# Eight weight slots of the second MLP combined early, sums on VectorE, and the first MLP's down layer turned to rows of tokens

## The reference

```python
kv  = einsum('bhsd,bhse->bhde', k, v); out = einsum('bhsd,bhde->bhse', q, kv)
x   = out / rms(out) * g_norm                       # 4608 tokens x 512
u   = x + real(fft(fft(x, axis=1), axis=2))         # first block
un  = (u - mean(u)) / sqrt(var(u) + 1e-6)
x   = u + relu(un @ w_ch1) @ w_ch2
u   = x + (xt @ U @ V) transposed back              # second block, rank 32
out = u + relu(u @ w_ch1b) @ w_ch2b
```

## Time and profile before

| | |
|---|---|
| median of 3 runs | 1830.46 us (1825.45 to 1831.49) |
| the profiled execution's own time | 1823.0 us |
| its span | 1820.9 us |
| TensorE matmul, busy | 1738.5 us (95%) |
| VectorE, busy | 1374.4 us (75%) |
| ScalarE, busy | 786.0 us (43%) |
| GpSimd, busy | 432.9 us (24%) |
| DMA, mean over the span | 258 GB/s |

### The profile page before, as it was taken

How to read it: one execution, slowest core, us unless ns; L and a number is a source line. 1 busy time by engine, 2 the same in 40 slices (tenths; PEclk the granted TensorE clock), 3 DMA queues, 4 the chain that set the end, 5 groups by cost and what they waited for, 6 DMA issues and landing times.

```text
span 1820.9 us, 25843 instructions
## 1 busy us (share of the span) xinstructions
PE 1738.5 (95%) x9908; PEld 1673.3 (92%) x9908; DVE 1374.4 (75%) x1631; ACT 786.0 (43%) x1126; POOL 432.9 (24%) x356
## 2 busy tenths in 40 slices
PE   6889879989999999999999999899999999999999
PEld 5667769979999999999999999799999999999999
DVE  5779987997777877867866858965956857758567
ACT  2333344554444544445444436434334434444442
POOL 2889973331120120120110013220110100100200
PEclk9889989999999999999999999999999999999999
DMA  8487557988787887887876778876766766767663
GB/s 256 161 272 250 201 201 282 370 332 283 262 303 261 283 287 258 289 286 247 297 260 232 257 246 310 333 275 231 251 236 237 257 234 242 255 231 254 224 249 128
DMA packets 123820, 470.04 MB, mean 258 GB/s; under 512 B 12274, under 2 KB 49650, under 8 KB 84019
## 3 DMA queue, kind: packets, MB, share of 16 engines
q1 hardware_dynamic: 122482, 467.21, 73.4%
q10 hardware_dynamic: 1216, 1.18, 0.2%
HBM read 389.70 MB, written 78.64 MB: 257 GB/s over the span
## 4 chain that ended last, share of the span: by engine, by line
PE 80%; DVE 12%; issue 3%; POOL 3%; DMA 2%; SPq 1%; ACT 0%; DVEq 0%; POOLq 0%; ACTq 0%
PE pair L832 12%; PE pair L834 12%; PE pair L833 12%; PE pair L849 12%; PE pair L851 12%; PE pair L850 12%; DVE t_lo L1339 2%; PE tr_ps L716 2%; PE pair L623 2%; DVE t_raw L1358 2%; DMA in_sb<-x_dram 1%; DVE w_sb L1271 1%; DMA v_sb<-v_rest 1%; DVE eo_sb L1229 1%; POOL x_sb L1528 1%
## 5 line engine op out<-in xcount | busy, mean ns | idle before, releaser
L849 PE MATMUL pair<-t_hi,w_sb 128*128 128x384 f32 x1344 | 460.4, 343 | 17.1 <-DVE t_lo L1339 16.7
L832 PE MATMUL pair<-t_hi,w_sb 128*128 128x384 f32 x1344 | 459.8, 342 | 7.0 <-DVE h_sb L1376 6.9
L851 PE MATMUL pair<-t_hi,w_sb 128*128 128x384 f32 x1344 | 456.9, 340 | 0.0
L850 PE MATMUL pair<-t_lo,w_sb 128*128 128x384 f32 x1344 | 456.8, 340 | 0.0
L833 PE MATMUL pair<-t_lo,w_sb 128*128 128x384 f32 x1344 | 455.1, 339 | 0.0
L834 PE MATMUL pair<-t_hi,w_sb 128*128 128x384 f32 x1344 | 455.0, 339 | 0.0
L1569 POOL TENSOR_TENSOR t_raw<-a_sb 128x768 f32<-128x768 f32 x60 | 126.1, 2103 | 920.1 <-PE pair L851 636.6
L1073 ACT ACTIVATE t_hi<-t_raw 128x768 fp32r<-128x768 f32 x240 | 202.6, 847 | 287.6 <-DVE t_raw L1358 287.6
L1339 DVE TENSOR_TENSOR t_lo<-t_raw,t_hi 128x768 fp32r<-128x768 f32 x300 | 306.7, 1028 | 12.9 <-ACT t_hi L1061 9.2
L849 PEld LDWEIGHTS pair<-t_hi,w_sb 128*128 128x128 f32 x1344 | 253.5, 189 | 23.8 <-DVE t_lo L1339 23.6
L832 PEld LDWEIGHTS pair<-t_hi,w_sb 128*128 128x128 f32 x1344 | 252.2, 188 | 14.3 <-issue 9.0
(11 more groups left out here) (148 smaller groups left out, 2005.3 us busy)
## 6 DMA issues: line engine op xcount, KB each, us to landing
w_sb<-wc SPq DMA_DIRECT2D x260, 1024.0 KB, 4.9
wc<-w_sb SPq DMA_DIRECT2D x28, 1024.0 KB, 5.7
w_raw<-wr1a SPq DMA_DIRECT2D x24, 512.0 KB, 5.1
w_raw<-wr1b SPq DMA_DIRECT2D x24, 512.0 KB, 4.3
wc<-pb SPq DMA_DIRECT2D x16, 640.0 KB, 4.8
w_raw<-wr2a SPq DMA_DIRECT2D x10, 1024.0 KB, 7.0
wc<-pb_v SPq DMA_DIRECT2D x16, 640.0 KB, 5.7
w_raw<-wr2b SPq DMA_DIRECT2D x10, 1024.0 KB, 7.2
```

Of the source, the lines that this page charges most:

```text
L832: nc.tensor.matmul(ps, w_hi, hi[:, x, :], start=(fresh and x == 0), stop=False, skip_group_check=True)
L849: nc.tensor.matmul(ps, w_hi, hi[:, f, :], start=(fresh and k == 0 and f == 0), stop=False, skip_group_check=True)
L850: nc.tensor.matmul(ps, w_hi, lo[:, f, :], start=False, stop=False, skip_group_check=True)
L851: last = nc.tensor.matmul(ps, w_lo, hi[:, f, :], start=False, stop=(k == 3 and f == 1), skip_group_check=True)
```

## The change

**Down layer of passes 0 to 5 (`g < NS`).** In `dn_step` the operands change places: 128 tokens of `hi` or `lo` are stationary and 256 columns of the weights move. A step is then 18 matmuls of 256 columns instead of 12 of 384, and the products lie in PSUM with tokens on the partitions. The evacuations write `ch_rows` (same bytes as `ch_sb`); `turn_out` and its semaphore are gone, and `add_residual` reads `ch_rows` from SBUF instead of PSUM.

**Slots of the second MLP.** The four products 5, 1, 7, 6 of the second MLP's down weights (8 slots) are combined beside passes 1 to 4, two a pass, as jobs through the bytes of `pb_v`. In pass 6 these 8 slots are loaded ready, like those of passes 7 to 11.

**Sums.** The sums of the 8 units of passes 1 to 4 and of the 8 jobs are VectorE's; before, GpSimd made the units' and those of the slots.

```diff
+AHEAD = (5, 1, 7, 6)
 def raw_slot(n):
     g, j = divmod(n, NSLOT)
-    return UP_SLOTS[j][0] not in STORED if j < len(UP_SLOTS) else g % NS == 0
+    if j < len(UP_SLOTS):
+        return UP_SLOTS[j][0] not in STORED
+    return g == 0 or g == NS and DN_SLOTS[j - len(UP_SLOTS)][0] not in AHEAD
...
+        JOBS = [(i, h) for i in AHEAD for h in range(2)]
+        JOB_AT = {(1 + x // 2, 16 + 28 * (x % 2)): x for x in range(len(JOBS))}
...
+            def load_job(x):            # SP, step t
+                sp.wait_ge(p_stored["v"], 32 * (x + 1))
+                sp.dma_start(job_raw..., wr2b[a:b + 1:b - a, h]...).then_inc(job_loaded, 16)
+            def store_job(x):           # SP, step t + 8
+                sp.wait_ge(job_lo, x + 1)
+                sp.dma_start(wc2[1][i - 1, h]..., job_sb...).then_inc(job_stored, 16)
...
+                if g < NS:
+                    for f in range(2):
+                        w_hi, w_lo = w[:, 0, 2 * (k % 2) + f, :, :], w[:, 1, 2 * (k % 2) + f, :, :]
+                        for c in range(CH):
+                            ps = pair[DN_PAIR[i]][:, 256 * c:256 * (c + 1)]
+                            cols = slice(128 * c, 128 * (c + 1))
+                            nc.tensor.matmul(ps, hi[:, f, cols], w_hi, ...)
+                            nc.tensor.matmul(ps, hi[:, f, cols], w_lo, ...)
+                            last = nc.tensor.matmul(ps, lo[:, f, cols], w_hi, ...)
...
                     if 1 <= g <= NS:
-                        if t in OUT_AT:
-                            tr_free(g, "out", NCH * (g - 1) + OUT_AT.index(t))
-                            turn_out(g - 1, OUT_AT.index(t))
                         if t in GATHER_AT:
                             gather(g - 1, GATHER_AT.index(t))
...
             def add_residual(g, j):
-                dve.wait_ge(out_turned, n + 1)
+                dve.wait_ge(dve_read, dve_count(g, "d7" if j < CH else "d6"))
+                dve.wait_ge(act_read, act_count(g, "d4" if j < CH else "d3"))
                 dve.wait_ge(res_loaded[j], 16 * (g + 1))
-                nc.vector.tensor_tensor(res_sb[j][:, :], tr_ps[:, :], res_sb[j][:, :], ALU.add)
+                nc.vector.tensor_tensor(res_sb[j][:, :], ch_rows[:, j, :], res_sb[j][:, :], ALU.add)
...
                     # VectorE's loop
+                    if (g, t - 4) in UNIT_AT:
+                        sum_unit(UNIT_AT[g, t - 4])
+                    if (g, t - 4) in JOB_AT:
+                        sum_job(JOB_AT[g, t - 4])
...
+                    if (g, t - 8) in JOB_AT:
+                        split_job_lo(JOB_AT[g, t - 8])
...
                     # GpSimd's loop
-                    if (g, t - 4) in UNIT_AT:
-                        sum_unit(UNIT_AT[g, t - 4])
```

More of the change, by code:

```diff
@@ L288, in both, with product @@
             return pair[n][:, :].rearrange("p (t n) -> p t n", t=2)[:, :, 0:TILE]
+        def product(g, i):
+            if g < NS:
+                return pair[DN_PAIR[i]][:, 0:CH * 256].rearrange("p (c n) -> p c n", c=CH)
+            return both(DN_PAIR[i])
         def sem(name):
@@ L509, in load_w @@
                         sp.wait_ge(p_stored[name], 32 * often)
+                if layer == 1 and n // NSLOT == NS:
+                    sp.wait_ge(job_stored, 16 * len(JOBS))
                 src = wc1[mlp][STORED.index(i), h] if layer == 0 else wc2[mlp][i - 1, h]
@@ L844, in dn_step @@
                 fresh = i in (1, 2, 5)
+                if g < NS:
+                    for f in range(2):
[3 more added lines that the diff above has]
+                            cols = slice(128 * c, 128 * (c + 1))
+                            nc.tensor.matmul(ps, hi[:, f, cols], w_hi, start=(fresh and k == 0 and f == 0 and c != 1), stop=False,
+                                             skip_group_check=True)
+                            nc.tensor.matmul(ps, hi[:, f, cols], w_lo, start=False, stop=False, skip_group_check=True)
+                            last = nc.tensor.matmul(ps, lo[:, f, cols], w_hi, start=False, stop=(k == 3 and f == 1),
+                                                    skip_group_check=True)
+                    last.then_inc(step, 1)
+                    return
                 for x in range(2):
@@ L864, in tr_free @@
                 first = q % NCH == 0
-                if what == "out":
-                    if first:
-                        pe.wait_ge(a_ready, NCH * (g + 1))
-                    else:
-                        pe.wait_ge(x2_ready, q)
-                elif what == "mix":
+                if what == "mix":
                     if g > NS:
@@ L883, in tr_free @@
                     pe.wait_ge(seq_copied, 8 * B)
-                elif first and g < NS:
-                    pe.wait_ge(x2_ready, NCH * g)
                 else:
@@ L1266, in split_unit_lo, with sum_unit, sum_job, split_job_lo @@
                                         ALU.subtract).then_inc(p_lo[name], 1)
+            def sum_unit(unit):
+                name, n = unit[:2]
+                dve.wait_ge(p_loaded[name], 16 * (n + 1))
+                raw = PB[name][1]
+                a11, a12, a21, a22 = [raw[:, 0, i, :] for i in range(4)]
+                nc.vector.tensor_tensor(raw[:, 1, 0, :], a11, a22, ALU.add)
+                nc.vector.tensor_tensor(raw[:, 1, 1, :], a21, a22, ALU.add)
+                nc.vector.tensor_tensor(raw[:, 1, 2, :], a11, a12, ALU.add)
+                nc.vector.tensor_tensor(raw[:, 1, 3, :], a21, a11, ALU.subtract)
+                nc.vector.tensor_tensor(raw[:, 1, 4, :], a12, a22, ALU.subtract).then_inc(p_summed[name], 1)
+            def sum_job(x):
+                dve.wait_ge(job_loaded, 16 * (x + 1))
+                a, b, op = slot_sum(job_raw, JOBS[x][0])
+                nc.vector.tensor_tensor(job_raw[:, 1, :, :, :], a, b, op).then_inc(job_summed, 1)
+            def split_job_lo(x):
+                dve.wait_ge(job_hi, x + 1)
+                nc.vector.tensor_tensor(job_sb[:, 1, :, :, :], job_raw[:, 1, :, :, :], job_sb[:, 0, :, :, :].bitcast(F32),
+                                        ALU.subtract).then_inc(job_lo, 1)
             def split_slot_lo(n):
@@ L1383, in read @@
                     dve.wait_ge(act_read, act_count(g, "d2"))
-                    nc.vector.tensor_tensor(ch_block("22"), ch_block("22"), both(DN_PAIR[5]), ALU.subtract).then_inc(dve_read, 1)
+                    nc.vector.tensor_tensor(ch_block(g, "22"), ch_block(g, "22"), product(g, 5), ALU.subtract).then_inc(dve_read, 1)
                 elif name == "d1":
@@ L1387, in read @@
                     dve.wait_ge(dve_read, dve_count(g, "d5"))
-                    nc.vector.tensor_tensor(ch_block("22"), both(DN_PAIR[1]), ch_block("22"), ALU.add).then_inc(dve_read, 1)
+                    nc.vector.tensor_tensor(ch_block(g, "22"), product(g, 1), ch_block(g, "22"), ALU.add).then_inc(dve_read, 1)
                 elif name in ("d4", "d3"):
@@ L1393, in read @@
                         dve.wait_ge(out_stored[block], 16 * (g - NS))
-                    nc.vector.tensor_tensor(ch_block(block), both(DN_PAIR[i]), a_block(g, block), ALU.add).then_inc(dve_read, 1)
+                    nc.vector.tensor_tensor(ch_block(g, block), product(g, i), a_block(g, block), ALU.add).then_inc(dve_read, 1)
                 else:
```

70 lines of the change are left out of this document (42 added, 28 removed).

## The result

The changed kernel takes 1806.32 us (median of 4 runs, 1804.23 to 1807.91) against 1829.88 us for the kernel before (4 runs, 1825.45 to 1831.49): a ratio of 0.9874 [0.9854, 0.9895], 23.6 us less. The prediction was 1809.0 us (21.5 less). On another chip the changed kernel took 1813.42 and 1815.24 us, and the kernel before 1834.26, 1836.16 and 1837.7, which is 19.0 to 24.3 us less.

What follows compares the result with a forecast made beforehand. TensorE was taken to pace passes 1 to 5 and 7 to 11, VectorE the down layers of 0 and 6. Terms +5.6 - 14.1 - 13.0 + 0 = -21.5 us from 1830.46 gave 1809.0 us, range 1796 to 1822.

Steps and rivals of the forecast that it cites:

- Change 1: Down step by rows of tokens: 18 matmuls of 256 columns at 0.120 us each; passes 1 to 5 cost +5.6 us.
- Both rivals on this step: Down step: short matmul cheaper, 0.112 us each, 1789 in all (chance 0.12); weight load shows, 0.148 each, 1880 (0.10).
- Change 2: Passes 0 to 5 without `turn_out`: 36 turns of 0.44 us go, 32 of them count, -14.1 us.
- Change 3: Pass 6's down layer: the eight slots' splits and GpSimd's sums no longer hold VectorE, -13.0 us.
- Change 4: Work added for VectorE beside passes 1 to 4: net 2.5 us against 7.9 us of down-layer pauses, so cost 0.
- VectorE bound of passes 1 to 4: Down layers of passes 1 to 4: pauses lie elsewhere than the new work, +2.5 us a pass, 1819 (chance 0.12).

Runs made afterwards that it cites:

- the rows alone: Changed kernel without early slots, every sum on GpSimd as before; down layer by rows of tokens, no `turn_out`: 1818.7 us (0.9942), run again 1816.57 us (0.9953).
- slots only: Changed kernel with the old down layer, `turn_out` and residual; only the eight jobs, pass 6's ready slots and VectorE's sums are new: 1814.45 us (0.9935).

## Why the prediction was right, and where it was not

The time was right (1806.3 for 1809.0), by two larger terms that held and by errors of 4 to 6 us that partly cancel. That the medians came so near is in part luck: for the profiled execution the prediction had 1801.5 us, and it took 1805.91.

- **Change 1, sized too high.** A step was to take 2.16 us, 0.120 a matmul; +5.6 us. Measured: 60.12 us for 28 steps and two turns of 0.44, so 2.116 a step and 0.1175 a matmul, the same as a step of 384 columns:

```profile
639.81 0.28 PE L889 MATMUL pair<-w_sb,t_hi 128*128 128x256 f32 x1
639.93 0.28 PE L891 MATMUL pair<-w_sb,t_hi 128*128 128x256 f32 x1
...
641.92 0.28 PE L889 MATMUL pair<-w_sb,t_hi 128*128 128x256 f32 x1
```

  These are 18 intervals in 2.11 us, from one step's start to the next. The line through 384 and 512 columns had given 0.118; the 0.002 that I added for "a small fixed part" was not in any row. The five down layers together are 0.3 us shorter in this profile and 1.8 and 0.8 us longer in the other two, where some take 60.63; the term had +5.6. The prediction named the spacing as the first sign of being wrong, and by its price (0.001 is 2.5 us) the miss is 6.3 us. Both rivals on this step fell: no 0.112, and the load doesn't show, though with 0.006 us a matmul to spare it was close.
- **Change 2 held.** All 36 turns went; the wait before step 19 went from 0.7 to 1.1 us each, as said. That -15.8 + 1.9 = -13.9 stands against the -14.1 of the sum, and the rows alone show 14.2 us over passes 1 to 6. The operation `add_residual`, whose two SBUF operands were to be priced "below with the locks" and never were, still took 0.68 us.
- **Change 3 held.** -13.1 us in the down layer for -13.0, alone (slots only) as together; with the other profiles of the kernel before it is -12.1 to -13.9. The longest wait for `t_lo` left in it is 0.2 us. The cause as well: VectorE pays mostly 2.2 us for a sum that GpSimd makes, shown by giving VectorE the sums: six of its own in place of five of GpSimd's, and the layer 3.6 us shorter. The page SBUF — State Buffer of the Trainium skill (section SBUF: two separate sides) has the rule of the exclusive lock; the runs agree (beside GpSimd's sum of 2.59 us an operation took 2.2 us longer). One thing was not in the sum: 1.0 us more in pass 6's up layer, where the wait for a reading fell from 1.8 to 0.8 us, with the slots alone too. Why is open: this wait varies by itself (1.4 and 2.1 us in other profiles of the kernel before, 1.3 in one of the changed), and it stays at 1.9 when VectorE makes pass 6's sums.
- **Change 4, the step that failed.** "In the up layer the job's sum falls between the layer norm of step 19 and the reading after step 20. So 0" looked only at the jobs. The units' five sums, which VectorE takes over at step 6 of the same layer, were not looked at: they and, in this profile, their late load put 3.6 us of waits in front of the gather. In the other two profiles these waits are 1.0 and 1.2 us; against the kernel with these sums on GpSimd the four up layers are 4.5 us longer here and 1.9 and 2.1 there. That the added work of the down layer costs nothing was right (no wait, 54.28 us of 60.12 busy). The rival "VectorE bound of passes 1 to 4" (+2.5 a pass) came near in size in pass 2 of this profile alone (2.2), and it looked at the wrong layer.
- **Pass 0** was to be within 1 us of 137.3; its down layer is (73.37 against 72.86), its up layer 4.0 us longer. Of this 2.2 us are waits (4.8 against 2.6) and 1.8 the clock (TensorE busy 63.57 against 61.81). It wasn't in the sum.
- **Passes 7 to 11** were taken as untouched; the wait for `in_sb` is 6.8 us in passes 7 to 10, where it was 5.2. The other profiles have 5.3 and 5.7 before and 6.3 and 5.1 after, so it isn't shown that the change raised it.

By passes 1 to 6 the measured sum is -24.2 us for -21.5: Change 1 gave 5.9 more, Change 4 took 3.6, pass 6's up layer gave 1.0; some 0.5 us of this account is not placed. The rest lies in passes 0 and 7 to 11, where executions differ by as much.

## What to carry to other kernels

Price a matmul of another width by the line through the widths that the trace has, and add nothing to it without a row; then ask separately whether its weight load still fits beneath. When work moves to an in-order engine, look at each place where it lands, in each layer, and at what stands behind it: a wait for a load there stops operations that have nothing to do with it, and a pause average of the whole pass says nothing about the place. Take more than one profile before you price such a wait: here it was 3.6 us in one and 1.0 and 1.2 in two others. A sum given to GpSimd isn't free for VectorE: where VectorE is the bound it is cheaper to make the sum itself or, better, not in that stage.
